# Attention beside the first MLP layer, in token tiles of 256 and 512, on one Trainium2 core

## The chip, the cores and the metric

One core of one Trainium2 chip runs one program. The time is device time in microseconds (us), from the start to the end of the program. Engines are named as in the profile: PE is TensorE (PEld its weight loads), DVE is VectorE, ACT is ScalarE, POOL is GpSimd, and SP is the engine that issues the DMAs.

## The reference

```python
# q, k, v: 4 batches x 8 heads x 576 positions x 64, float32
scores = scale * np.matmul(q, k.transpose(0, 1, 3, 2))
mask = block_i >= block_j            # blocks of 64 positions, causal by block
scores = np.where(mask, scores, -1e9)
attn = np.exp(scores - max) / (sum + 1e-9)
x = (attn @ v) as 2304 tokens x 512
h = x @ w_in;  x = (h * sigmoid(h)) @ w_out            # layer 1: 512 -> 2048 -> 512
h = x @ w_in2; y = (h * sigmoid(1.702 * h)) @ w_out2   # layer 2
```

All is float32. Products of the MLP and the scores are made of three matmuls each: an operand is split into a high part (rounded to fp32r) and a low part (the rest), and lo*hi, hi*hi and hi*lo are summed.

## The kernel before

**Attention** works on 16 head pairs (two heads are one pair; a batch has four pairs). A pair has nine rows, one for each block of 64 queries of both heads; row s has 576 - 64 s keys, the longest first. `scores` (L357 to 373) makes a row with three matmuls, DVE takes its maximum (L643), ACT its exp with the sum (L521), DVE adds 1e-9 to the sums (L602), inverts them (L607) and multiplies the rows (L616). `transposes` (L375 to 392) turns the rows in eight batches into PSUM, which ACT (L496) and DVE (L596) copy out as `pt_sb`; `pv` (L394 to 410) multiplies by v, and `take_pv` (L632) stores the result in `x_f`. The loop holds three pairs at once: rows of pair n, transposes of n - 1, values of n - 2. Operands are prepared ahead: SP loads q, k and v; POOL scales q (L311); ACT makes `k_hi` and `q_hi` (L503, L509); POOL makes `k_lo` (L315) and `q_lo` (L321).

**MLP.** Tokens are cut into three tiles of 768 and both layers run as six tiles of 16 chunks (128 of the 2048 hidden channels each), 96 chunks. `hidden(c)` (L432) makes a chunk's 128 hidden channels, for 512 and then for 256 tokens: 24 matmuls; ACT takes the sigmoid (L554), DVE the product (`gate`, L693), ACT and DVE its high and low part (L561, L697), and `output(c)` (L449) adds the chunk's share to 512 output channels: 24 matmuls. PE issues `hidden(c + 1)` ahead of `output(c)`. The weights of a chunk, 512 KB, are loaded by SP into a ring of two (`w_raw`, L250 to 253) and split by POOL into a ring of four (`w_hi` L329, `w_lo` L331); the split of chunk c waits until `output(c - 4)` is done. ACT and DVE split the next tile's x (L550, L686) and take a tile's output from PSUM (L563, L700).

**Order.** Each engine runs its own list of instructions in program order, and semaphores tie the lists together. All attention comes first; `hidden(0)` sits among the transposes of the last pair (L478 to 482), and the 96 chunks follow (L485). Scores and hidden sums share the four PSUM banks `ps_s`; transposes, values and output sums share `ps_y`.

Of the kernel before, what the change touches and what calls it, by code (L numbers as in the profile page):

```python
# [30 lines left out]
PAIRS = B * H // 2  # L31
# [7 lines left out]
QA = 4  # L39
# [15 lines left out]

GROUPS = [(0, 1), (1, 3), (3, 5), (5, 7), (7, 9)]

SUMS_AT = {1: (4, True), 2: (0, False), 4: (1, False), 6: (2, False), 8: (3, False)}
# [8 lines left out]
TT = 768  # L67
MAIN = 512
SIDE = TT - MAIN
NT = TOK // TT  # L70
NTILES = 2 * NT
NCHUNK = NTILES * NF
RING = 4
ALPHA = (1.0, 1.702)


def build(nc, qT, kT, v_main, v_tail, w_chunks, out):
    ctx = ExitStack()
    with ctx:
# [3 lines left out]
        def sb(stack, name, shape, dt=F32):  # L83
            return stack.enter_context(nc.sbuf_tensor(name, shape, dt))


        x_f = sb(ctx, "x_f", [P, NK * TOK])
        w_hi = sb(ctx, "w_hi", [P, RING, CW], F32R)
        w_lo = sb(ctx, "w_lo", [P, RING, CW], F32R)
        w_raw = sb(ctx, "w_raw", [P, 2, CW])  # L90
        ident = sb(ctx, "ident", [P, P])
        x_hi0 = sb(ctx, "x_hi0", [P, NK, TT], F32R)
        x_lo0 = sb(ctx, "x_lo0", [P, NK, TT], F32R)

        att = ExitStack()
        q_raw = sb(att, "q_raw", [P, 2, S])
        k_raw = (sb(att, "k_raw0", [P, S]), sb(att, "k_raw1", [P, S]))
        q_hi = sb(att, "q_hi", [P, 2, NQ, 2, BLK], F32R)
        q_lo = sb(att, "q_lo", [P, 2, NQ, 2, BLK], F32R)
        scale_sb = sb(att, "scale_sb", [P, S])  # L100
        k_hi = sb(att, "k_hi", [P, 2, S], F32R)
        k_lo = sb(att, "k_lo", [P, 2, S], F32R)
        v_sb = sb(att, "v_sb", [P, 2, NJ, P])
        p_sb = sb(att, "p_sb", [P, 2, PCOLS])

        pt_sb = sb(att, "pt_sb", [P, 2, PT_BLOCKS * P])
        pt_last = sb(att, "pt_last", [P, 2, P])
# [114 lines left out]
        def tokens_of(t):  # L222

            return (t % NT) * TT

# [536 lines left out]
```

## Time and profile before

| what | us |
|---|---|
| median of 3 runs (1039.07 to 1040.92) | 1039.37 |
| profiled execution, its own time | 1041.74 |
| profiled execution, span from first to last instruction | 1040.0 |
| PE busy | 998.6 (96%) |
| PE weight loads busy | 850.5 (82%) |
| DVE busy | 407.0 (39%) |
| ACT busy | 338.8 (33%) |
| POOL busy | 422.3 (41%) |

The profile is of one execution, by the hardware profiler. Busy time is the union of the times of an engine's instructions; PE's weight loads overlap its matmuls, and the ends of matmuls are modelled, so steps between their starts say more than their durations. In the page's 40 slices of 26 us, PE is 50 to 90% busy in the first nine and 90% or more in the rest; DVE goes from 70 to 90% to about 20% at the same place. Of a wait for several semaphores, the profile names the one that came last.

### The profile page before, as it was taken

Reading aid. Unit: us, or ns where it says so; the run is one execution under the profiler, and the core shown is the slowest. Engines: PE = TensorE matmul, PEld = TensorE weight load, DVE = VectorE, ACT = ScalarE, POOL = GpSimd, SP = SyncE. Lnnn points to the kernel's source line nnn. Section 1 sums busy time; section 2 is a strip of 40 time slices with the busy share of each in tenths; the row PEclk is TensorE's granted clock in tenths of the full one; section 3 lists DMA queues with packets and bytes.
Section 4 is the critical chain, followed back from the end, with each engine's and each line's share of the span. In section 5 each row is a group of like instructions: output and inputs, shape, how many; then the busy total and the mean of one; then the engine's idle time right before and its main releaser. Section 6 shows DMA issues by size and latency. Waiting matters only on the chain.

```text
span 1040.0 us, 15291 instructions
## 1 busy us (share of the span) xinstructions
PE 998.6 (96%) x5936; PEld 850.5 (82%) x5936; DVE 407.0 (39%) x777; ACT 338.8 (33%) x652; POOL 422.3 (41%) x261
## 2 busy tenths in 40 slices
PE   5898888889999999999999999999999999999998
PEld 4666666668888888888888888888888888888887
DVE  7978888962222222222322222222232322222222
ACT  5767766652222122222222212222122221212222
POOL 6434443522444444443344444444333444443330
PEclk9989999999999999999999999999999999999999
DMA  4212221030221111112221111111223111131201
GB/s 154 81 46 68 68 68 57 23 101 29 69 69 61 62 61 61 61 61 64 71 70 61 61 61 62 61 61 61 70 72 122 61 61 61 61 122 63 66 34 61
DMA packets 24244, 69.96 MB, mean 67 GB/s; under 512 B 2688, under 2 KB 4224, under 8 KB 24192
## 3 DMA queue, kind: packets, MB, share of 16 engines
q1 hardware_dynamic: 24192, 69.22, 20.6%
q8 instruction: 39, 0.64, 0.3%
q14 instruction: 13, 0.11, 0.0%
HBM read 64.49 MB, written 4.72 MB: 67 GB/s over the span
## 4 chain that ended last, share of the span: by engine, by line
PE 89%; DVE 7%; issue 3%; DVEq 0%; DMA 0%; ACT 0%
PE ps_s L444 13%; PE ps_s L445 13%; PE ps_s L446 13%; PE ps_y L460 8%; PE ps_y L461 8%; PE ps_y L462 8%; PE ps_s L471 4%; PE ps_s L470 4%; PE ps_s L468 4%; PE ps_y L390 4%; PE ps_y L406 4%; PE ps_s L370 4%; DVE den_e L602 2%; DVE nmax L643 2%; DVE p_sb L616 2%
## 5 line engine op out<-in xcount | busy, mean ns | idle before, releaser
L329 POOL CAST w_hi<-w_raw 128x1024 fp32r<-128x1024 f32 x96 | 104.5, 1088 | 472.7 <-PE ps_s L471 452.0
L693 DVE TENSOR_TENSOR g_f<-ps_s,sig 128x768 f32<-128x768 f32 x96 | 91.9, 958 | 497.2 <-ACT sig L554 497.2
L444 PE MATMUL ps_s<-x_hi,w_lo 128*128 128x512 f32 (+1 forms) x768 | 258.9, 337 | 2.5 <-DVE x_f L636 1.5
L445 PE MATMUL ps_s<-x_hi,w_hi 128*128 128x512 f32 (+1 forms) x768 | 259.2, 337 | 0.0
L446 PE MATMUL ps_s<-x_lo,w_hi 128*128 128x512 f32 (+1 forms) x768 | 258.1, 336 | 0.0
L554 ACT ACTIVATE sig<-ps_s 128x768 f32<-128x768 f32 x96 | 78.0, 812 | 503.2 <-PE ps_s L446 503.2
L331 POOL TENSOR_TENSOR w_lo<-w_raw,w_hi 128x1024 fp32r<-128x1024 f32 x96 | 229.8, 2394 | 7.7
L444 PEld LDWEIGHTS ps_s<-x_hi,w_lo 128*128 128x128 f32 x768 | 145.8, 190 | 19.1 <-DVE x_f L636 1.6
L446 PEld LDWEIGHTS ps_s<-x_lo,w_hi 128*128 128x128 f32 x768 | 145.5, 189 | 15.7
L445 PEld LDWEIGHTS ps_s<-x_hi,w_hi 128*128 128x128 f32 x768 | 145.8, 190 | 15.1
L460 PE MATMUL ps_y<-g_hi,w_lo 128*128 128x512 f32 x384 | 150.6, 392 | 0.0
L461 PE MATMUL ps_y<-g_hi,w_hi 128*128 128x512 f32 x384 | 150.6, 392 | 0.0
L462 PE MATMUL ps_y<-g_lo,w_hi 128*128 128x512 f32 x384 | 149.4, 389 | 0.0
L697 DVE TENSOR_TENSOR g_lo<-g_f,g_hi 128x768 fp32r<-128x768 f32 x96 | 92.0, 959 | 87.7 <-ACT g_hi L561 87.7
L561 ACT ACTIVATE g_hi<-g_f 128x768 fp32r<-128x768 f32 x96 | 81.3, 847 | 105.4 <-DVE g_f L693 105.4
L471 PE MATMUL ps_s<-g_lo,w_hi 128*128 128x256 f32 x384 | 108.7, 283 | 0.0
L470 PE MATMUL ps_s<-g_hi,w_hi 128*128 128x256 f32 x384 | 108.6, 283 | 0.0
L468 PE MATMUL ps_s<-g_hi,w_lo 128*128 128x256 f32 x384 | 108.2, 282 | 0.0
L390 PEld LDWEIGHTS ps_y<-ident,p_sb 128*128 128x128 f32 x400 | 46.3, 145 | 59.6 <-DVE pt_last L596 29.2
L390 PE MATMUL ps_y<-ident,p_sb 128*128 128x128 f32 x400 | 72.2, 294 | 23.1 <-DVE pt_last L596 22.8
L521 ACT ACTIVATE p_sb<-ps_s,nmax 128x576 f32<-128x576 f32 (+2 forms) x144 | 75.2, 527 | 41.7 <-DVE nmax L643 41.1
L462 PEld LDWEIGHTS ps_y<-g_lo,w_hi 128*128 128x128 f32 x384 | 72.1, 188 | 15.7
(58 smaller groups left out, 1206.5 us busy)
## 6 DMA issues: line engine op xcount, KB each, us to landing
w_raw<-w_chunks SPq DMA_DIRECT2D x96, 512.0 KB, 3.4
q_raw<-qT SPq DMA_DIRECT2D x16, 288.0 KB, 2.9
k_raw<-kT SPq DMA_DIRECT2D x16, 288.0 KB, 3.1
v_sb<-v_main SPq DMA_DIRECT2D x16, 256.0 KB, 2.5
yT<-x_f SPq DMA_DIRECT2D x2, 1536.0 KB, 7.5
yT<-x_f SPq DMA_DIRECT2D x6, 256.0 KB, 2.1
v_sb<-v_tail SPq DMA_DIRECT2D x16, 32.0 KB, 2.4
```

Source lines behind the costliest of these rows:

```text
L329: nc.gpsimd.tensor_copy(w_hi[:, c % RING, :], w_raw[:, c % 2, :]).then_inc(s_whi, 1)
L331: nc.gpsimd.tensor_tensor(w_lo[:, c % RING, :], w_raw[:, c % 2, :], w_hi[:, c % RING, :].bitcast(F32), ALU.subtract).then_inc(s_w, 1)
L390: last = nc.tensor.transpose(ps_y[:, col:col + P], p_sb[:, par, a:a + P], ident[:, :])
L444: nc.tensor.matmul(dst, lo[:, w], x_hi[t % 2][:, k, a:b], start=(k == 0), stop=False)
L445: nc.tensor.matmul(dst, hi[:, w], x_hi[t % 2][:, k, a:b], start=False, stop=False)
L446: last = nc.tensor.matmul(dst, hi[:, w], x_lo[t % 2][:, k, a:b], start=False, stop=(k == NK - 1))
L460: nc.tensor.matmul(dst, lo[:, w], g1[:, 0:MAIN], start=(f == 0), stop=False)
L461: nc.tensor.matmul(dst, hi[:, w], g1[:, 0:MAIN], start=False, stop=False)
L462: last = nc.tensor.matmul(dst, hi[:, w], g2[:, 0:MAIN], start=False, stop=(f == NF - 1))
L468: nc.tensor.matmul(dst, lo[:, w], g1[:, MAIN:TT], start=(f == 0 and k % 2 == 0), stop=False, skip_group_check=True)
L470: nc.tensor.matmul(dst, hi[:, w], g1[:, MAIN:TT], start=False, stop=False, skip_group_check=True)
L471: last = nc.tensor.matmul(dst, hi[:, w], g2[:, MAIN:TT], start=False, stop=(f == NF - 1), skip_group_check=True)
```

## The change

Attention and the first MLP layer are laid beside each other in all five lists.

- **Tiles.** `LAYER` cuts the tokens into one tile of 256 and four of 512; the second layer takes the four of 512 first and the one of 256 last. There are 160 chunks. x_hi, x_lo, g and the PSUM banks have 512 columns; `ps_h` (hidden, one bank), `ps_a` (attention, three banks) and `ps_y` (output, four banks) are apart.
- **Early part.** The first 256 positions of batch 0 (rows of four blocks, four pairs) are computed first, one pair after the other, with `ps_y` for scores. They are what the first tile needs. The 16 jobs that follow each have rows 4 to 8 of pair n (the upper 320 positions) and, for the first 12 (`FULL`), the four short rows of pair n + 4. The last four have five rows.
- **Windows.** `AT` gives the chunk beside which a job's rows are computed: -1, 3, 7, 11, 14, 18, ... 58. In that chunk PE's list has the rows between pieces of three matmuls of `hidden(c + 1)` and `output(c)`, placed by `WIDE_ROWS` or, beside 256-token chunks, `SLIM_ROWS`. The values of the job before stand at the end of the window's chunk, the job's transposes at the ends of the next two or three chunks. DVE has maxima, two additions, and four multiplications ahead of the window's `gate(c + 1)`; ACT has all exps ahead of the window's sigmoid.
- **Preparation.** In chunk AT + 1 POOL scales the next job's q, at the end of AT + 2 ACT makes its `k_hi` and `q_hi` (`prepare`), and then POOL makes `k_lo` and `q_lo`. A job's buffers p_sb, pt_sb, nmax, den are single, not double.
- **x.** `split_high` and `split_low` make a quarter of the next tile's x behind the values of each job (`PV_AT`).
- **Weights.** POOL splits chunk c + 3 in its step c, now 160 times; in the last tile's chunks (`c >= LAST`) ACT makes the high part and POOL the low part only.

The core of the diff:

```diff
-TT = 768
-MAIN = 512
-SIDE = TT - MAIN
-NT = TOK // TT
-NTILES = 2 * NT
+LAYER = [(0, 256), (256, 512), (768, 512), (1280, 512), (1792, 512)]
+TILES = LAYER + LAYER[1:] + LAYER[:1]
+NTILES = len(TILES)
...
+AT = [-1, 3, 7, 11] + [14 + 4 * n for n in range(JOBS - PER)]
+WINDOW = {c: n for n, c in enumerate(AT)}
+WIDE_ROWS = (0, 0, 3, 3, 3, 4, 5, 5, 6)
+SLIM_ROWS = (0, 0, 4, 4, 5, 7, 7, 8, 8)
+PV_AT = {c: n - 1 for n, c in enumerate(AT) if n}
...
+PREP_AT = {AT[n] + 2: n + 1 for n in range(JOBS - 1)}
+SCALE_AT = {AT[n] + 1: n + 1 for n in range(JOBS - 1)}
...
+            for c in range(-1, NCHUNK):
+                if c + 3 < NCHUNK:
+                    if c + 3 < LAST:
+                        chunk_high(c + 3)
+                    chunk_low(c + 3)
+                if c in SCALE_AT:
+                    scale_q(SCALE_AT[c])
+                if c in PREP_AT:
+                    keys_low(PREP_AT[c])
+                    queries_low(PREP_AT[c])
...
+            for c in range(NCHUNK):
+                n = WINDOW.get(c)
+                before = WIDE_ROWS if TILES[c // NF][1] == TMAX else SLIM_ROWS
+                for piece in range(2 * NK + 1):
+                    if n is not None:
+                        for s in range(rows_of(n)):
+                            if before[s] == piece:
+                                scores(n, s)
+                    if piece < NK:
+                        if c + 1 < NCHUNK:
+                            hidden(c + 1, piece)
+                    elif piece < 2 * NK:
+                        output(c, piece - NK)
+                if c in PV_AT:
+                    values(PV_AT[c], True, n)
+                    if PV_AT[c] < FULL:
+                        values(PV_AT[c], False, n)
+                if c in TRANSPOSE_AT:
+                    for bt in TRANSPOSE_AT[c][1]:
+                        transposes(TRANSPOSE_AT[c][0], bt)
...
+            for c in range(-1, NCHUNK - 1):
+                t, f = c // NF, c % NF
+                if f == 0 and t:
+                    take_output(t - 1)
+                if c > 0 and c in WINDOW:
+                    for s in range(rows_of(WINDOW[c])):
+                        exp_row(WINDOW[c], s)
+                sigmoid(c + 1)
+                g_high(c + 1)
...
+                if c in PREP_AT:
+                    prepare(PREP_AT[c])
...
+                if LAST <= c + 3 < NCHUNK:
+                    chunk_high(c + 3)
...
+                    for s in range(0 if n else 4, min(6, rows_of(n))):
+                        row_max(n, s)
+                    add_guard(n, 0)
+                    if n < FULL:
+                        row_max(n, 6)
+                    invert(n, 0)
+                    multiply(n, 0)
+                    if n < FULL:
+                        row_max(n, 7)
+                        row_max(n, 8)
+                    multiply(n, 1)
+                    multiply(n, 2)
+                    add_guard(n, 1)
+                    invert(n, 1)
+                    multiply(n, 3)
+                    gate(c + 1)
+                    if c in PV_AT:
+                        take_upper(PV_AT[c])
+                    g_low(c + 1)
```

## Rows read from the trace of the kernel before

**Rows 1.** Busy time by engine: attention, MLP, tail (PEclk is the granted clock).

```profile
7.95:237.98 230.03, 199.92 (x1353) 145.77 (x1353) 191.52 (x544) 152.44 (x419) 97.99 (x67) 0.97 0.22 67
237.98:1036.62 798.64, 798.64 (x4584) 704.66 (x4584) 210.29 (x227) 181.98 (x228) 320.12 (x184) 1.00 0.20 65
1036.62:1040.00 3.38, 0.00 (x1) 0.00 (x0) 0.69 (x1) 0.00 (x0) 0.00 (x0) 1.00 0.73 256
```

Columns: from:to, length, then busy us (and instructions) of PE, PEld, DVE, ACT and POOL, granted clock, DMA share, GB/s.

**Rows 2.** The page's chain that ended last, by engine.

```profile
PE 89%; DVE 7%; issue 3%; DVEq 0%; DMA 0%; ACT 0%
```

**Rows 3.** Busy time by engine over one head pair in mid-attention.

```profile
99.77:113.19 13.42, 11.60 (x85) 8.32 (x84) 11.75 (x33) 9.28 (x27) 5.71 (x4) 1.00 0.22 66
```

**Rows 4.** Timeline of PE in `hidden(0)`: start, duration, engine, line, operation.

```profile
225.60 0.40 PE L444 MATMUL ps_s<-x_hi,w_lo 128*128 128x512 f32 x1
...
227.65 0.28 PE L444 MATMUL ps_s<-x_hi,w_lo 128*128 128x256 f32 x1
...
228.96 0.28 PE L446 MATMUL ps_s<-x_lo,w_hi 128*128 128x256 f32 x1
```

**Rows 5.** Instructions by line and shape, DVE in attention: busy us, mean ns, idle before.

```profile
L616 DVE TENSOR_SCALAR p_sb<-p_sb,rden 128x192 f32<-128x192 f32 x16 | 21.2, 1322 | 0.0
...
L643 DVE TENSOR_REDUCE nmax<-ps_s 128x1 f32<-128x256 f32 x16 | 6.4, 402 | 1.2 <-PE ps_s L370 1.2
...
L616 DVE TENSOR_SCALAR p_sb<-p_sb,rden 128x256 f32<-128x256 f32 x16 | 5.5, 343 | 0.0
...
L616 DVE TENSOR_SCALAR p_sb<-p_sb,rden 128x64 f32<-128x64 f32 x16 | 3.9, 243 | 0.0
```

**Rows 6.** The same view: ACT's batch copy and keys, POOL's low parts.

```profile
L496 ACT ACTIVATE pt_sb<-ps_y 128x512 f32<-128x512 f32 x80 | 47.4, 592 | 32.7 <-PE ps_y L390 32.7
...
L321 POOL TENSOR_TENSOR q_lo<-q_raw,q_hi 64x576 fp32r<-64x576 f32 x30 | 43.1, 1435 | 2.7
...
L315 POOL TENSOR_TENSOR k_lo<-k_raw,k_hi 128x576 fp32r<-128x576 f32 x15 | 21.4, 1424 | 100.4 <-ACT k_hi L503 99.7 <-DVE k_lo L667 0.7
...
L503 ACT ACTIVATE k_hi<-k_raw 128x576 fp32r<-128x576 f32 x16 | 11.0, 688 | 1.1 <-DMA k_raw<-kT 1.1
```

**Rows 7.** Timeline of DVE and POOL from 101 us.

```profile
101.04 0.68 DVE L643 TENSOR_REDUCE nmax<-ps_s 128x1 f32<-128x512 f32 x1
...
101.36 2.96 POOL L321 TENSOR_TENSOR q_lo<-q_raw,q_hi 64x576 fp32r<-64x576 f32 x2
...
101.64 1.15 DVE L602 TENSOR_SCALAR den_e<-den 128x2 f32<-128x2 f32 x1
...
102.70 1.73 DVE L616 TENSOR_SCALAR p_sb<-p_sb,rden 128x256 f32<-128x256 f32 x2
```

**Rows 8.** Instructions by line, POOL's split of a weight chunk.

```profile
L329 POOL CAST w_hi<-w_raw 128x1024 fp32r<-128x1024 f32 x96 | 104.5, 1088 | 472.7 <-PE ps_s L471 452.0
...
L331 POOL TENSOR_TENSOR w_lo<-w_raw,w_hi 128x1024 fp32r<-128x1024 f32 x96 | 229.8, 2394 | 7.7
```

**Rows 9.** Timeline of ACT: its two table loads, and the first sigmoid.

```profile
0.74 1.28 ACT L532 ACT_TABLE_LOAD   x1 [0.74 <-PEq L756]
...
232.23 1.28 ACT L554 ACT_TABLE_LOAD   x1
...
233.52 0.81 ACT L554 ACTIVATE sig<-ps_s 128x768 f32<-128x768 f32 x1
```

**Rows 10.** DMA issues of the page: KB each, us to landing.

```profile
w_raw<-w_chunks SPq DMA_DIRECT2D x96, 512.0 KB, 3.4
```

**Rows 11.** Busy time and granted clock of two stretches of 4 us.

```profile
46.00:50.00 4.00, 2.19 (x16) 1.40 (x15) 4.00 (x11) 1.51 (x5) 2.88 (x3) 1.00 0.32 86
50.00:54.00 4.00, 4.00 (x23) 2.55 (x21) 2.64 (x11) 3.16 (x10) 0.00 (x0) 0.64 0.17 66
```

**Rows 12.** Timeline of POOL and DVE at the start.

```profile
5.39 1.79 POOL L311 TENSOR_TENSOR q_raw<-q_raw,scale_sb 128x576 f32<-128x576 f32 x1 [2.12 <-DMA q_raw<-qT]
...
5.96 1.84 DVE L667 TENSOR_TENSOR k_lo<-k_raw,k_hi 128x576 fp32r<-128x576 f32 x1
```

More of the change, by code:

```diff
@@ L95, in build @@
[L95 to L104, printed above, removed]
@@ L412, in pair @@
-            def pair(n, par, it, cur=True, prev=True, prev2=True, also=None):
-                for s in range(NQ):
-                    if cur:
-                        scores(n, par, it, s)
-                    if prev2:
-                        for part in MULTIPLY.get(s, ()):
-                            pv(n - 2, par, it - 1, part)
-                    if prev and s in TRANSPOSE:
-                        transposes(n - 1, 1 - par, TRANSPOSE[s])
-                    if also and s in also:
-                        also[s]()
@@ L478, in first_hidden @@
[L478 to L488 removed]
+            early_transposes(0)
+            early_scores(2)
@@ new lines, in _ @@
+            early_transposes(1)
+            early_values(0)
+            early_scores(3)
+            early_transposes(2)
+            early_values(1)
+            early_transposes(3)
+            scores(0, 0)
+            scores(0, 1)
+            early_values(2)
+            early_values(3)
+            scores(0, 2)
+            scores(0, 3)
+            for k in range(NK):
+                hidden(0, k)
+                scores(0, 4 + k)
+            scores(0, 8)
+            pe.wait_ge(s_pad, 1)
@@ L578, in _ @@
-            act.wait_ge(s_xe, 2 * H)
-            pair(PAIRS, 0, PAIRS // 2, cur=False, ahead=False, also={k: (lambda k=k: split_x(0, k)) for k in range(NK)})
-            for c in range(NCHUNK):
+                    nc.scalar.activation(x_kt[:, k, a:a + w], bank_y(k)[:, 0:w], ACT.Copy).then_inc(s_ea, 1)
+            for a in range(2):
+                early_high(a)
+            early_exp(0)
+            early_high(2)
+            early_exp(1)
+            early_high(3)
+            early_take(0)
@@ new lines, in _ @@
+            for r in range(LB):
+                early_multiply(PER - 1, r)
+            early_take(3)
+            row_max(0, 0)
+            early_values(2)
+            row_max(0, 1)
+            split_low(0, 0)
+            split_low(0, 1)
+            early_values(3)
+            for i in range(LB, NQ, 2):
+                last = nc.vector.memset(p_sb[:, POFF[i] + BLK * (i + 1):POFF[i] + PAD[i]], 0.0)
+            last.then_inc(s_pad, 1)
+            row_max(0, 2)
+            split_low(0, 2)
```

1026 lines of the change are left out of this document (602 added, 424 removed).

## The prediction

> **What bounds the kernel now.** I first read the stretches [rows 1]. Of a span of 1040.0 us, TensorE (PE) is busy 199.92 in the 230.03 us of attention and all 798.64 in those of the two MLP layers. The reader is to see two regimes: from 237.98 on nothing but less work for PE can shorten the kernel; before that some 30 us of PE idle time are to be had, beside the 7.95 us ahead of its first matmul. Then the chain that ended last [rows 2]: 89% PE, 7% DVE. Then one head pair in the middle of attention [rows 3]: of 13.42 us PE is busy 11.60, DVE 11.75, ACT 9.28, POOL 5.71. Attention is a relay among four engines in which DVE and PE are both nearly full. In the MLP stretch DVE, ACT and POOL are busy 26%, 23% and 40%: room for attention, and PE's idle time would be filled by matmuls.
>
> **PE's work after the change.** A 512-column matmul takes (227.65 - 225.60)/9 = 0.228 us, a 256-column one (228.96 - 227.65)/11 = 0.119 [rows 4]. Before, each of 96 chunks has 24 of each: 8.33 us, 800 in all. After, 128 chunks have 24 of 512 columns (5.48 us) and 32 have 24 of 256 (2.86): 792.8 us, 7.4 less, since fewer narrow matmuls are issued. A pair costs 11.6 us [rows 3], of which 4.6 are scores and 3.6 values by the steps between their starts. I keep 11.6 between MLP matmuls; the lower bound is 10.8, without the gaps of 0.15 to 0.2 us at changes of kind, worth 13 us over 16 pairs; the upper one 11.6, as that includes all gaps.
>
> **Head, up to `hidden(1)`.** The four early jobs go through a serial chain: scores, maximum, exp, sums, multiply, transpose, take, values. Per job DVE has four maxima (0.402 for 256 columns), four multiplications (0.24 to 0.34 [rows 5]), low parts, sums, two copies: 4.6 us, plus waits for each exp; from a first score at 6 us the four end near 27. Then job 0's nine rows, the splits of x, and 4 multiplications stand ahead of `gate(0)`: `hidden(1)` at 40 us. PE does 4 x 3.4 us for the early jobs and 6.4 for job 0 meanwhile. Bounds 34 and 47 us (each early job 1.5 us shorter or longer).
>
> **Rest of PE's work.** 16 x 11.6 = 185.6, less 13.6 and 6.4, is 166 us; MLP 792.8 less `hidden(0)` is 791.4; the tail 3.4 us [rows 1], 3.2 with copies of 256. Without any stall: 40 + 166 + 791.4 + 3.2 = 1000.6. The kernel can give away 39 us before it is level, so what counts is the hand-offs.
>
> **Operands of the next job late.** At the end of chunk AT+2 ACT takes batch 4 (0.59), then makes k_hi (0.69 for 576 columns, 0.96 for the 832 of a wide job); then POOL makes k_lo (1.42, so 2.05) and q_lo (2 x 1.44) [rows 6]. With hand-overs of 0.4 in all that is 6.9 us from the end of PE's chunk AT+2 to the next job's first score. PE has one chunk meanwhile. In the 256-token tile that is 2.86 + 0.6 of transposes: a stall of 3.5, three times. Job 4 is prepared in chunk 13 and its window is 14: 6.8 us. With 512 tokens PE has 6.1: 0.8, seven times. The last four jobs have shorter operands: none. Sum 17.3 + 5.6 = 22.9; bounds 12 and 30 (chain shorter or longer by a third of a chunk).
>
> **DVE behind POOL.** POOL starts two q_lo subtractions at 101.36; DVE's addition on two numbers per partition, issued at 101.64, takes 1.15 us, and the next two multiplications 1.73, until POOL is done [rows 7]. The means say the same: 192 columns take 1.322 us, 256 columns 0.343 [rows 5]. So a DVE op from SBUF to SBUF waits for POOL's op to end; the reduction from PSUM at 101.04 does not (0.68). Ahead of `gate(c+1)`, on which `hidden(c+2)` waits, DVE now has two such additions and four multiplications. In a 512-token window I lay the rows end to end: PE ends the last score at 8.7 us, the output at 10.0 (5.48 + 4.6) and the values at 13.7; DVE ends its multiplications at 10.9, ACT its last exp at 9.5 and the sigmoid at 11.4, and the gate ends at 12.3. POOL's chunk (1.09 + 2.39 [rows 8]) lies before 7 us or after 10. Slack 1.4 us: 3 us over eleven windows. In the 256-token tile POOL comes out of q_lo two chunks in arrears and works through the multiplications without pause; six ops meet parts of 2.39 us ops, and the gate comes some 3 us after PE: 4 x 3 = 12. Together 15; bounds 0 (DVE always gets in first) and 15 windows x 2.39 = 36.
>
> **Activation tables.** Exp and Sigmoid are a load of 1.283 us apart, so thirty more loads [rows 9]. The load to Exp falls where ACT idles: the first one ran at 0.74, ahead of the wait for its data. The load to Sigmoid stands behind the window's last exp (9.5 to 10.8 above): hidden by the 1.4 us of slack, price 0.
> In the trace the sigmoid starts 0.01 us after its load (232.23 + 1.28, 233.52). The Trainium skill (ScalarE: Activation LUTs, What ACT_TABLE_LOAD costs) speaks against the change: a drain of 1380 ns comes with each switch, 2.66 us in all. By it, as an estimate from that page, each sigmoid would come 1.4 us later and the sum would rise by 0 to 10 us; the trace shows no such drain, so none is taken.
>
> **x split at tile borders.** `hidden` of chunks 16, 32 and 48 needs the last job's x, which DVE splits only behind all multiplications of the window: 2.5 + 2.9 + 2.9 = 8.3 by the same laying end to end; bounds 0 and 12.
>
> **Last tile.** Landing 3.4 us [rows 10], the cast now on ACT about 1.08 (1024 columns by the slope of its copies [rows 6]), w_lo 2.39, hand-overs 0.2: 7.1 us around a ring of two slots, 3.5 per chunk where PE wants 2.86. Over some 11 chunks 7.5 us; ACT can't run on the four buffers' lead, as the cast waits in its queue ahead of the next sigmoid. Bounds 0 (lead used) and 12.
>
> **Clock.** After 4 us with PE busy 2.19, the granted clock was 0.64 for the next 4 [rows 11]: 1.4 us lost. Four stalls of 3.5 to 7 us may each bring the lower of the two levels (1.2 instead of 2.4 GHz). I take 2 us in all; bounds 0 and 8.
>
> **SP's queue.** Windows put q, k and v loads between chunk loads; chunk loads run two chunks ahead of POOL's need, which hides them. Price 0; if that cover goes, one landing, 3.4 us, per window.
>
> **Sum.** 1000.6 + 22.9 + 15 + 8.3 + 7.5 + 2 = 1056.3 us of span. The profiled execution took 1041.74 with its span of 1040.0; the median of the runs is 1039.37, 0.6 below that span. So 1056 us, 1.6% slower.
>
> **Rivals.** 1, the other side: the hand-offs in chunks 0 to 15 are absorbed. Place: windows 3, 7, 11, 14 and their gates. Price: 17.3 for late operands and 12 for POOL's hold on DVE, with them the clock's 2, and 6 of the last tile if its lead is used: 1056 - 37 = 1019. It decides where all stalls together stay below 39. For it: the 256-column multiplication at 102.70 did get in between two POOL ops. Against it: the chain of 6.9 us is made of plain durations. Chance 0.28.
> 2, worse: DVE is also held in the 512-token windows, and not in its multiplications alone, but in subtractions of two SBUF operands (`g_low`, `split_low`): at 5.96 such a k_lo took 1.84 us beside POOL's scaling [rows 12]. One 2.39 us op more in some nine windows: 1056 + 22 = 1078. Chance 0.14.
> The Trainium skill (SBUF — State Buffer, SBUF: two separate sides) states the hold for both kinds of operation, as an exclusive lock; by that rule, the trace agrees.
> 3, the change does less than it says: attention runs beside the MLP, but parts of each stall give the gain back to the level of before, within 2 us of 1039. Chance 0.04.
>
> **Numbers.** Forecast 0.54, with 1044 to 1068 as its own range. The whole range takes in rival 1's value and rival 2's: 1020 to 1078. A measurement of this kernel tells some 0.2% from no change. Faster 0.28, same 0.04, slower 0.68.
>
> **What would show it.** `hidden(1)` near 40 us; chunk 16 at 165 (126 us for 94 of PE work); chunk 62 at 551; then 5.48 us per chunk; chunks 144 to 159 at 3.5. Scores at chunks 3, 7, 11, 14 wait for q_lo, and multiplications there average over 1 us. I am wrong if PE is over 97% busy between 40 and 551 us, or if the last tile runs at 2.86 per chunk.

## The result, and the profile after

The kernel after takes 1061.14 us (median of 4 runs, 1057.68 to 1065.3), the one before 1039.22 beside it (1038.38 to 1040.92). The ratio is 1.0211, with a 95% interval of 1.017 to 1.0251: slower by 22 us where 17 were forecast. The profiled execution took 1057.68 us with a span of 1055.7; it is the fastest of the four. Medians are of executions that took the usual time: one of the kernel before (1966.74 us) and one of the run with four edits together (5532.26 us) are left out.

First the page of the kernel after: busy time by engine, then the chain that ended last, by engine [rows 2].

```profile
PE 985.9 (93%) x5168; PEld 825.6 (78%) x5168; DVE 466.1 (44%) x878; ACT 422.4 (40%) x837; POOL 649.8 (62%) x386
...
PE 80%; POOL 7%; DVE 6%; ACT 3%; DMA 2%; issue 2%; POOLq 0%; DVEq 0%
```

The chain had no POOL before; now 7% of it is POOL, which makes operands that PE waits for. Next the stretches of the kernel after, cut where `hidden(1)` starts, at chunks 16 and 62, and ahead of the last tile, with the columns of [rows 1].

```profile
0.00:54.20 54.20, 31.61 (x157) 25.50 (x158) 39.26 (x88) 23.81 (x75) 29.52 (x31) 0.84 0.41 130
54.20:181.90 127.70, 99.66 (x717) 91.89 (x716) 75.55 (x164) 63.59 (x146) 77.47 (x47) 0.91 0.31 104
181.90:552.90 371.00, 361.86 (x1961) 294.31 (x1959) 199.51 (x397) 188.63 (x374) 227.97 (x137) 1.00 0.27 91
552.90:997.80 444.90, 444.90 (x1969) 368.74 (x1970) 132.06 (x196) 119.07 (x198) 281.62 (x160) 1.00 0.30 102
997.80:1055.70 57.90, 47.90 (x373) 45.19 (x371) 19.67 (x34) 27.33 (x47) 33.25 (x14) 1.00 0.41 144
```

Against the forecast, stretch by stretch. The forecast's column is added from the prediction's terms, without its 2 us for the clock, for which it gives no place:

| stretch | forecast | measured | difference |
|---|---|---|---|
| up to `hidden(1)` | 40 | 54.2 | +14.2 |
| chunks 0 to 15 | 126 | 127.7 | +1.7 |
| chunks 16 to 61 | 385.7 | 371.0 | -14.7 |
| chunks 62 to 143 | 448.1 | 444.9 | -3.2 |
| last tile and tail | 55.0 | 57.9 | +2.9 |

The span came out 0.6 us from the forecast's 1056.3 because two errors of some 14 us cancel; that closeness is luck. PE idles 22.6 us in the first stretch, 28.0 in the second, 9.1 in the third, none in the fourth and 10.0 in the fifth. What it waited for, in the whole trace after: total, times, longest.

```profile
PE ps_a L557 <- POOL q_lo L428: 20.9, 11, 6.0
PE ps_a L513 <- DVE p_sb L850: 14.5, 7, 4.9
PE ps_h L620 <- DVE g_f L908: 9.6, 4, 2.9
PE ps_h L620 <- POOL w_lo L443: 6.5, 9, 1.2
PE ps_y L498 <- POOL k_lo L408: 5.2, 1, 5.2
PE ps_h L620 <- DVE x_lo L900: 3.3, 2, 2.4
PE ps_h L620 <- issue: 2.8, 1, 2.8
```

The reader is to see the forecast's terms by name. Late operands are the first line (15.6 of it in four waits in chunks 0 to 15, 5.3 in seven of at most 0.8 later). DVE behind POOL, ahead of the gate, is the third and the last: three waits of 2.9 us in the windows of chunks 3, 7 and 11, and the 2.8, which is the same wait in the window of chunk 14 (DVE's gate ended at 175.30, 0.1 us ahead of the matmul at 175.40). The fourth wait of that third line, 1.0 us up to 53.95, belongs to the head: PE waits there for `gate(0)`. The last tile is the fourth. The second, DVE's multiplications in the early jobs (L850), was in no term.

DVE by form, with the columns of [rows 5]: in chunks 0 to 15 of the kernel after the multiplication of 512 columns, then `g_low` and `gate` in chunks 16 to 61, then `g_low` behind them:

```profile
L882 DVE TENSOR_SCALAR p_sb<-p_sb,rden 128x512 f32<-128x512 f32 x4 | 9.0, 2243 | 0.0
...
L913 DVE TENSOR_TENSOR g_lo<-g_f,g_hi 128x512 fp32r<-128x512 f32 x47 | 48.1, 1023 | 25.1 <-ACT g_hi L758 25.1
...
L908 DVE TENSOR_TENSOR g_f<-ps_h,sig 128x512 f32<-128x512 f32 x46 | 31.7, 690 | 82.3 <-ACT sig L750 82.3
...
L913 DVE TENSOR_TENSOR g_lo<-g_f,g_hi 128x512 fp32r<-128x512 f32 x81 | 56.1, 692 | 56.6 <-ACT g_hi L758 56.6
```

A multiplication of 512 columns takes 2.24 us in the first tile and 0.48 later. `g_low`, with both operands in SBUF, takes 1.02 us beside attention and 0.69 without; `gate`, of the same size with an operand in PSUM, takes 0.69 in both. One instance of each, begun while POOL was at work:

```profile
207.14 2.38 POOL L443 TENSOR_TENSOR w_lo<-w_raw,w_hi 128x1024 fp32r<-128x1024 f32 x1
...
208.53 1.53 DVE L913 TENSOR_TENSOR g_lo<-g_f,g_hi 128x512 fp32r<-128x512 f32 x1
...
225.35 3.45 POOL L428 TENSOR_TENSOR q_lo<-q_raw,q_hi 64x576 fp32r<-64x576 f32 x2
225.45 0.69 DVE L908 TENSOR_TENSOR g_f<-ps_h,sig 128x512 f32<-128x512 f32 x1 [3.04 <-ACT sig L750]
```

That `gate` simply never met POOL can be ruled out in the same trace. Of its operations of 512 columns in chunks 16 to 143, 84 began inside a running operation of POOL, with 0.19 to 1.35 us of it to go, and each took 0.69. Of the 46 of `g_low` in chunks 16 to 61, the 20 that began inside one, with 0.73 to 0.99 us of it to go, took 1.28 to 1.54; the other 26 took 0.69. Behind chunk 61 `g_low` began inside none, which is why it takes 0.69 there.

One window of the first tile in the kernel after, in the timeline:

```profile
68.06 0.40 PE L557 MATMUL ps_a<-k_hi,q_lo 128*128 128x288 f32 x1 [3.51 <-POOL q_lo L428]
...
77.72 2.44 POOL L443 TENSOR_TENSOR w_lo<-w_raw,w_hi 128x1024 fp32r<-128x1024 f32 x1
...
78.20 3.75 DVE L882 TENSOR_SCALAR p_sb<-p_sb,rden 128x512 f32<-128x512 f32 x2
...
80.25 0.38 ACT L750 ACTIVATE sig<-ps_h 128x256 f32<-128x256 f32 x1
...
82.61 0.42 DVE L908 TENSOR_TENSOR g_f<-ps_h,sig 128x256 f32<-128x256 f32 x1
...
83.17 0.55 PE L620 MATMUL ps_h<-x_hi,w_lo 128*128 128x256 f32 x1 [2.87 <-DVE g_f L908]
```

Both forecast waits are here: 3.51 us for the operands (3.5 forecast), and 2.87 for the gate (3 forecast). The sigmoid was done at 80.6; the gate came 2 us later because two multiplications took 3.75 us between POOL's operations.

### The profile page after: what moved, and what is told of

Read it like the earlier page. It is cut to its first block, busy times and chain, and to the rows that moved or that the text cites. A ratio compares the mean times of both kernels' runs of the same rounds, so it can differ in the third digit from the quotient of the medians.

```text
span 1055.7 us, 13667 instructions
## 1 busy us (share of the span) xinstructions
PE 985.9 (93%) x5168; PEld 825.6 (78%) x5168; DVE 466.1 (44%) x878; ACT 422.4 (40%) x837; POOL 649.8 (62%) x386
## 4 chain that ended last, share of the span: by engine, by line
PE 80%; POOL 7%; DVE 6%; ACT 3%; DMA 2%; issue 2%; POOLq 0%; DVEq 0%
PE ps_h L620 12%; PE ps_h L621 11%; PE ps_h L622 11%; PE ps_y L636 11%; PE ps_y L638 11%; PE ps_y L637 11%; PE ps_a L557 6%; POOL q_lo L428 3%; PE ps_a L602 3%; PE ps_a L579 3%; POOL k_lo L420 2%; DMA w_raw<-w_chunks 2%; DVE p_sb L882 2%; DVE p_sb L850 1%; POOL w_lo L443 1%
## 5 line engine op out<-in xcount | busy, mean ns | idle before, releaser
L443 POOL TENSOR_TENSOR w_lo<-w_raw,w_hi 128x1024 fp32r<-128x1024 f32 x160 | 386.2, 2414 | 39.6 <-ACT w_hi L763 28.0
L620 PE MATMUL ps_h<-x_hi,w_lo 128*128 128x512 f32 (+1 forms) x640 | 244.0, 381 | 22.2 <-DVE g_f L908 9.6
L622 PE MATMUL ps_h<-x_lo,w_hi 128*128 128x512 f32 (+1 forms) x640 | 237.9, 372 | 0.0
L636 PE MATMUL ps_y<-g_hi,w_lo 128*128 128x512 f32 (+1 forms) x640 | 237.4, 371 | 0.5 <-DVE g_lo L913 0.5
L621 PE MATMUL ps_h<-x_hi,w_hi 128*128 128x512 f32 (+1 forms) x640 | 237.8, 371 | 0.0
L638 PE MATMUL ps_y<-g_lo,w_hi 128*128 128x512 f32 (+1 forms) x640 | 236.2, 369 | 0.0
L637 PE MATMUL ps_y<-g_hi,w_hi 128*128 128x512 f32 (+1 forms) x640 | 236.0, 369 | 0.0
L913 DVE TENSOR_TENSOR g_lo<-g_f,g_hi 128x512 fp32r<-128x512 f32 (+1 forms) x160 | 126.1, 788 | 95.6 <-ACT g_hi L758 95.2
L620 PEld LDWEIGHTS ps_h<-x_hi,w_lo 128*128 128x128 f32 x640 | 122.9, 192 | 46.9 <-issue 14.8
L621 PEld LDWEIGHTS ps_h<-x_hi,w_hi 128*128 128x128 f32 x640 | 123.0, 192 | 18.9
L636 PEld LDWEIGHTS ps_y<-g_hi,w_lo 128*128 128x128 f32 x640 | 121.3, 190 | 20.2 <-DVE g_lo L913 0.7
L557 PE MATMUL ps_a<-k_hi,q_lo 128*128 128x288 f32 (+8 forms) x144 | 47.8, 332 | 22.8 <-POOL q_lo L428 20.9
```

Source lines behind the costliest of these rows:

```text
L443: nc.gpsimd.tensor_tensor(w_lo[:, c % RING, :], w_raw[:, c % 2, :], w_hi[:, c % RING, :].bitcast(F32), ALU.subtract).then_inc(s_w, 1)
L557: last = nc.tensor.matmul(dst, q_part[:, par, i, :, :].rearrange("p h c -> p (h c)"), k_part[:, par, a:a + width], start=(q_part is q_lo), ...
L620: nc.tensor.matmul(dst, lo, x_hi[:, t % 2, k, 0:w], start=(k == 0), stop=False)
L621: nc.tensor.matmul(dst, hi, x_hi[:, t % 2, k, 0:w], start=False, stop=False)
L622: last = nc.tensor.matmul(dst, hi, x_lo[:, t % 2, k, 0:w], start=False, stop=(k == NK - 1))
L636: nc.tensor.matmul(dst, lo, g_hi[:, c % 2, 0:w], start=(f == 0), stop=False)
```

## The experiments

All times of stretches below come from the first instruction of a chunk's sigmoid on ACT in the timeline: from the start of the span to that of chunk 1, then to 16, to 63, to 144, and from there to the end of the span. A run's median is the time of the kernel as a whole.

```
                          median   0-1    1-16   16-63  63-144  144-end
after                     1061.1   55.7   124.1  376.1  439.4   60.5
multiplications on ACT    1054.4   50.5   124.2  378.0  439.4   60.4
operands one earlier      1049.4   55.2   114.0  378.4  439.4   60.2
three raw slots           1054.6   55.9   123.2  377.7  439.3   56.7
gate ahead                1073.2   55.7   138.0  378.3  439.4   60.2
exp for sigmoid           1060.5   54.8   129.7  377.7  439.4   60.5
slots and cast first      1056.2   55.5   128.3  378.0  439.3   53.2
matmuls in the head       1065.3   55.1   126.7  378.0  439.4   64.5
three together            1040.0   49.2   112.0  378.4  439.3   56.7
four together             1034.8   50.4   112.1  378.4  439.3   52.1
sums first                1033.6   48.9   112.7  378.4  439.4   52.0
x split moved             1030.8   47.0   112.1  378.4  439.3   52.0
```

**The early multiplications on ACT.** Sixteen operations leave DVE.

```diff
-            def early_multiply(a, r):
-                if r == 0:
-                    dve.wait_ge(s_eden, 2 * a + 2)
-                nc.vector.tensor_scalar(e_probs(a, r), e_probs(a, r), e_rden[:, a, r:r + 1], None,
-                                        ALU.mult).then_inc(s_enm, 1)
...
+            def early_multiply(a):
+                act.wait_ge(s_eden, 2 * a + 2)
+                for r in range(LB):
+                    nc.scalar.activation(e_probs(a, r), e_probs(a, r), ACT.Copy,
+                                         scale=e_rden[:, a, r:r + 1]).then_inc(s_enm, 1)
```

> The sixteen multiplications of the early part move from DVE to ACT; nothing else changes. Theory (DVE is held by POOL's ops): the change's head lasts 54 us instead of the 40 forecast, and its DVE multiplications took 0.6 to 2.3 us each where 0.24 to 0.34 is their own time; ACT is not held, so the head shortens by about 10 us and the kernel with it (1061 to about 1051). Rival (the head is a serial relay at the lower clock): ACT's multiplications are each a little longer than DVE's own, so the head stays within 2 us of 54 and the kernel within 2 us.

Measured: 1054.4 us, ratio 1.0138 (1.0097 to 1.0179); the sigmoid of chunk 1 starts at 50.5 us instead of 55.7. In the kernel after, DVE and POOL in the head (timeline):

```profile
15.60 2.34 POOL L443 TENSOR_TENSOR w_lo<-w_raw,w_hi 128x1024 fp32r<-128x1024 f32 x1
...
15.86 2.20 DVE L850 TENSOR_SCALAR p_sb<-p_sb,e_rden 128x192 f32<-128x192 f32 x1
...
27.89 2.34 POOL L443 TENSOR_TENSOR w_lo<-w_raw,w_hi 128x1024 fp32r<-128x1024 f32 x1
...
27.95 2.33 DVE L850 TENSOR_SCALAR p_sb<-p_sb,e_rden 128x64 f32<-128x64 f32 x1
...
34.10 4.74 DVE L850 TENSOR_SCALAR p_sb<-p_sb,e_rden 128x256 f32<-128x256 f32 x4
```

Even 64 columns take 2.33 us, and end with POOL's operation. With them on ACT, PE's wait there is 5.7 us in three, for ACT's batch copies, in place of 14.5. So the hold is real in the head too, but this way gave 5 us of the 10 expected: a relay was behind it (below). The four executions of this run lie 8.6 us apart, so the stretch (5.2 us) says more than the total (6.7).

**Operands one chunk earlier.**

```diff
-PREP_AT = {AT[n] + 2: n + 1 for n in range(JOBS - 1)}
-SCALE_AT = {AT[n] + 1: n + 1 for n in range(JOBS - 1)}
+PREP_AT = {AT[n] + 1: n + 1 for n in range(JOBS - 1)}
+SCALE_AT = {AT[n]: n + 1 for n in range(JOBS - 1)}
```

> Scaling q and preparing the next job's operands stand one chunk earlier in POOL's and ACT's lists (AT and AT + 1 instead of AT + 1 and AT + 2). Theory (late operands): PE's waits for q_lo ahead of a job's scores, 15.6 us in chunks 0 to 15 and 5.3 us later, go; with the lower clock behind them, 15 to 22 us less: about 1042. Rival (POOL is the bound of the 256-token tile, 3.5 us a chunk and 6.4 a job): the wait only moves to the weight split or to the gates, and the kernel stays within 5 us of 1061.

Measured: 1049.39 us, ratio 1.009 (1.0073 to 1.0107), 12 us less, between the 15 to 22 of the theory and the 5 of the rival. PE's waits in its trace:

```profile
PE ps_a L557 <- DVE pt_sb L887: 7.3, 10, 1.3
PE ps_h L620 <- DVE g_f L908: 7.2, 4, 2.6
...
PE ps_a L602 <- ACT p_sb L725: 5.1, 3, 1.8
...
PE ps_a L557 <- POOL q_lo L428: 1.3, 1, 1.3
```

The wait for q_lo fell from 20.9 to 1.3 us. In chunks 1 to 16 that gave 10.1 us. There the wait for q_lo had been 15.6, but PE's idle time fell by 7.2 only (28.0 to 20.8), as waits for ACT's exps (5.1) and a weight split (1.7) came in its place; the other 3 us are PE's matmuls, busy 93.2 instead of 96.1 us at a granted clock of 0.96 instead of 0.90. In chunks 16 to 63 it gave nothing, since the ten waits of 7.3 us for DVE's batch copies took the place of the 5.3 that left.

**Three slots for the raw weights.** `w_raw` and its semaphores get three slots instead of two; SP waits for `s_w` two chunks back instead of one.

```diff
-                if c >= 2:
-                    sp.wait_ge(s_w, c - 1)
+                if c >= RAW:
+                    sp.wait_ge(s_w, c - RAW + 1)
```

> The ring for unsplit weights gets a third slot, the loads run one chunk further ahead. Theory (the last tile goes round a two-slot ring of landing, ACT cast and POOL low part, 7.1 us for two chunks): chunks 144 to 159 go from 3.55 to about 2.9 us, 8 to 10 us less: about 1052; the layers between stay at 5.44 us a chunk. Rival (the cast in ACT's list, between the high part of g and the next sigmoid, sets the pace): the last tile stays at 3.4 us or more per chunk, and the kernel within 2 us of 1061.

Measured: 1054.57 us, ratio 1.0126 (1.0098 to 1.0155). PE's wait for w_lo in the last tile of the kernel after stands above (6.5 us in nine); ACT's for the landing there:

```profile
ACT w_hi L763 <- DMA w_raw<-w_chunks: 6.9, 11, 1.8
```

With three slots ACT's cast waits for no transfer there, and PE for POOL only this much (L621 and L444 are the L620 and L443 of the kernel after):

```profile
PE ps_h L621 <- POOL w_lo L444: 2.0, 7, 0.3
```

The last stretch is 3.8 us shorter, 3.29 us per chunk (between the sigmoids of 145 and 159) instead of 3.56. So the landing was part of the ring, as forecast, but the 2.9 us expected did not come: it did not set the pace alone.

**Three slots, and the cast ahead of the sigmoid.** The rest of that ring was ACT's cast, which stands behind sigmoid and g_high.

```diff
+                if LAST <= c + 3 < NCHUNK:
+                    chunk_high(c + 3)
                 sigmoid(c + 1)
                 g_high(c + 1)
...
-                if LAST <= c + 3 < NCHUNK:
-                    chunk_high(c + 3)
```

> The raw ring of three, and in the last tile ACT's cast of chunk c + 3 stands ahead of the sigmoid of c + 1 instead of behind the high part of g. With the ring alone the last tile went from 3.55 to 3.29 us a chunk. Theory (what is left is the way cast, then POOL's low part 2.40, then the hidden matmuls two chunks on, begun 2 us too late): 2.9 us a chunk, 5 us less than with the ring alone, about 1049. Rival (POOL's low part and the loads' landing set 3.3): no change from the ring alone, 1054.

Measured: 1056.18 us, ratio 1.0136 (1.0101 to 1.0171): by the total, no gain over three slots alone. By the stretches there is one: 53.2 us instead of 56.7, and 2.91 us per chunk, PE's own pace. In this profiled execution chunks 1 to 16 took 5.1 us more, which the edit does not touch (see the clock, below). The total, where 1049 was expected, hid a gain that the stretch shows.

**The gate ahead of the multiplications** in the windows of the first tile.

```diff
+                elif n and t == 0:
+                    for s in range(rows_of(n)):
+                        row_max(n, s)
+                    gate(c + 1)
+                    take_upper(PV_AT[c])
+                    g_low(c + 1)
+                    take_lower(PV_AT[c])
+                    for g in range(3):
+                        add_guard(n, g)
+                        invert(n, g)
+                        for s in range(3 * g, 3 * g + 3):
+                            multiply(n, s)
```

> In the four windows of the 256-token tile DVE does the nine maxima, then the gate, the copies of the values and the low part of g, and only then the additions, inversions and multiplications. Theory (DVE is held by POOL in multiplications that stand ahead of the gate): PE's 9.6 us of waits for g_f in these windows go, and the kernel is about 8 us shorter: 1053. Rival (the sigmoid is late, behind nine exps and a table load): the waits stay, now behind the sigmoid, and the multiplications, now later, delay the transposes: within 2 us of 1061 or slower.

Measured: 1073.21 us, ratio 1.0315 (1.0297 to 1.0332), 12 us slower than the kernel after. The timeline of this run at the window shown above, and at the gate behind it:

```profile
80.53 0.36 PE L620 MATMUL ps_h<-x_hi,w_lo 128*128 128x256 f32 x1 [0.16 <-DVE g_f L908]
...
84.03 3.65 DVE L882 TENSOR_SCALAR p_sb<-p_sb,rden 128x384 f32<-128x384 f32 x3
...
89.76 0.56 PE L620 MATMUL ps_h<-x_hi,w_lo 128*128 128x256 f32 x1 [5.13 <-DVE g_f L908]
```

The wait of 2.87 us is gone, and one of 5.13 stands at the next gate, behind the same multiplications. Between the sigmoids of chunks 1 and 16 PE idles 37.1 us instead of 28.0; the other 4.8 us of the 13.9 lost are PE's own, busy 100.9 instead of 96.1 at a granted clock of 0.86 instead of 0.90. DVE's held time did not become slack in this order.

**Exp in the place of Sigmoid beside attention.** Up to chunk 59 the kernel computes exp(h) where the reference has a sigmoid, so no table is loaded there.

```diff
-                nc.scalar.activation(sig[:, 0:w], ps_h[:, 0:w], ACT.Sigmoid,
+                nc.scalar.activation(sig[:, 0:w], ps_h[:, 0:w], ACT.Exp if c <= AT[-1] + 1 else ACT.Sigmoid,
```

> In chunks 0 to 59, beside attention, ACT applies Exp where it applied Sigmoid, so the thirty activation table loads between them go; the kernel computes another function there, all else is the same. Theory (the loads lie in idle time of ACT or within slack): at most 4 us less than 1061, nearly all in the 256-token tile. Rival (each load costs its 1.28 us, or 2.66 with a drain, on the path to the gate): 15 windows, so 15 to 35 us less.

Measured: 1060.48 us, ratio 1.0184 (1.0163 to 1.0205), against 1061.14 and 1.0211. ACT's table loads in the kernel after, and below them those of this run:

```profile
L750 ACT ACT_TABLE_LOAD x16 | 20.5, 1283 | 0.3
...
L725 ACT ACT_TABLE_LOAD x15 | 19.2, 1283 | 0.3
```

```profile
L750 ACT ACT_TABLE_LOAD x1 | 1.3, 1283 | 0.0
```

Thirty loads, 38.5 us of ACT's time, cost the kernel nothing that can be told: the sigmoid of the window above started at 78.98 instead of 80.25 us, and the gate still had to wait for DVE. In the windows with 512 tokens the window's sigmoid comes 1.4 us earlier and the next one not at all: from chunk 22's to 23's and on to 24's the steps are 13.51 and 6.69 us, and 14.94 and 5.27 in the kernel after, 20.2 both times. That is the slack that the forecast counted on.

**Matmuls in the head.** Ninety matmuls of 256 columns are added, whose results nothing reads, so that PE does not idle in the early jobs.

```diff
+            def fill(a, count):
+                if a == 3 and count:
+                    pe.wait_ge(s_exe, 1)
+                for _ in range(count):
+                    nc.tensor.matmul(ps_h[:, 0:LT] if a == 3 else bank(2)[:, 0:LT],
+                                     q_hi[:, 1, 0, :, :].rearrange("p h c -> p (h c)"),
+                                     k_hi[:, 1, 0:LT], start=True, stop=True)
+            FILL = {(1, 6): 16, (1, 7): 6, (2, 6): 12, (2, 7): 18, (3, 6): 36, (3, 7): 2}
...
+                    fill(a, FILL.get((a, bt), 0))
```

> Ninety matmuls of 256 columns into a PSUM bank that nobody reads are put where PE waits in the early part (ahead of the transposes of early jobs 1 to 3); about 10 us of PE work at 2.4 GHz, in waits of 13 us. Theory (the lower clock is half of the head's lateness: granted 0.84 over 0 to 54 us, and the scores and values of each early job are links of the serial chain): clock near 1.00 and hidden(1) 4 to 7 us earlier. Rival (DVE's and POOL's operations set the head, PE's speed doesn't): hidden(1) within 1 us of 54.2, or later by what the filling delays.

Measured: 1065.26 us, ratio 1.0221 (1.0188 to 1.0254). Two stretches of the head in the kernel after, and the same two with the matmuls:

```profile
30.00:38.00 8.00, 2.78 (x13) 1.67 (x14) 5.69 (x8) 0.00 (x0) 7.71 (x6) 0.50 0.17 66
38.00:46.00 8.00, 7.00 (x32) 4.65 (x31) 3.24 (x7) 1.90 (x5) 0.59 (x1) 0.55 0.01 3
```

```profile
30.00:38.00 8.00, 7.18 (x61) 6.50 (x59) 6.11 (x8) 0.00 (x0) 7.77 (x6) 0.99 0.19 66
38.00:46.00 8.00, 6.78 (x38) 4.87 (x36) 3.96 (x9) 2.42 (x7) 0.79 (x1) 0.79 0.02 4
```

The granted clock rose from 0.50 to 0.99 and from 0.55 to 0.79, and the sigmoid of chunk 1 came only 0.6 us earlier, as the rival had it. So the lower clock in the early jobs goes with the long head and does not make it. It was not lifted everywhere: job 0's first scores ran at the lower level with the matmuls too (0.50 from 41.5 to 43.0 us; 512-column steps of 0.43 us, for the 0.228 worked out from [rows 4]), and what that costs was not tried. The total is 4 us above that of the kernel after because of stretches that the edit does not touch: the last took 64.5 us instead of 60.5, with 9.3 us of waits for w_lo instead of 6.5.

**Three together** (multiplications on ACT, operands earlier, three slots).

> The early multiplications on ACT, operands prepared one chunk earlier and the raw ring of three, together. Theory (three separate losses, one behind another in time): the gains of the single runs add, 1061 - 7 - 12 - 6 = about 1036, level with or just below the kernel before. Rival (they stand on one resource, POOL, and each cure shifts wait to the next): less than half of the sum, 1048 or more.

Measured: 1040.01 us (10 runs, 1037.9 to 1040.42), ratio 0.9989 (0.9979 to 1.0). The three alone took 6.7, 11.8 and 6.6 us off 1061.14, together 21.1 of their 25.1. The stretches, less noisy, say the same: 5.2 in the head, 10.1 in chunks 1 to 16 and 3.8 in the last, each alone, and 6.5, 12.1 and 3.8 together. So the waits are largely separate, and the change without them is level with the kernel before.

**Four together**, with the cast ahead of the sigmoid, and **the sums first** in the early jobs:

```diff
+                early_sums(a)
                 if a >= 2:
                     early_values(a - 2)
-                early_sums(a)
                 if a:
                     early_take(a - 1)
```

> The three edits of the run before it (multiplications of the early jobs on ACT, operands prepared one chunk earlier, three raw slots for the weights) and the fourth, the last tile's cast of chunk c+3 ahead of the sigmoid of chunk c+1. Theory: in the trace with three slots the stretch from the sigmoid of chunk 144 to the end took 56.7 us, with the cast ahead of the sigmoid 53.2, though the total of that run did not show it, as the stretches before it were slower there; so 3.5 us less than the 1040.0 of the three together, 1036.5 us, ratio to the kernel before 0.9955 to 0.9975, and 2.9 us per chunk in the last tile. Rival: the cast holds up ACT's sigmoids by as much as it gains, the two runs of the last tile agree in their totals because nothing was gained: 1040 us, ratio 0.999.

> The four edits, and in the early jobs DVE's sum and reciprocal stand ahead of its copy of the values of two jobs before, instead of behind it. In the trace of the three together ACT finished the exponentials of the third early job at 18.5 us, but its multiplications began at 21.35, since DVE waited 3.85 us for the values of an earlier job, that copy being ahead of the sum in its queue; so again at 26.4. Theory: what made the head longer than forecast is this order, a relay in which each early job waits for the values of an earlier one: 2.3 us less for each of two early jobs, some 4.5 in all, first sigmoid at 42 us instead of 46.5, total 1032 us, ratio about 0.992. Rival: POOL's operands for the first full job (its last subtraction ended at 27.6 us) or its weight splits set the head: the first sigmoid stays above 45 us and the total within 1.5 us of the run with four edits.

Measured, four together: 1034.77 us, ratio 0.9934 (0.9922 to 0.9947); the last stretch took 52.1 us, so here the cast shows in the total as well. Sums first: 1033.64 us, ratio 0.9926 (0.9913 to 0.9939), 1.1 less where 4.5 were expected; chunk 1's sigmoid came 1.5 us earlier. The first sigmoid, that of chunk 0, came at 44.9 us, neither at 42 nor above 45, and the total is the rival's. DVE's last early batch copy and the x splits in the timeline of three together, then of sums first:

```profile
31.46 0.42 DVE L860 COPY pt_sb<-ps_a 128x256 f32<-128x256 f32 x1 [3.28 <-PE ps_a L514]
...
37.40 2.60 DVE L905 TENSOR_TENSOR x_lo<-x_f,x_hi 128x256 fp32r<-128x256 f32 x2
```

```profile
25.90 0.42 DVE L859 COPY pt_sb<-ps_a 128x256 f32<-128x256 f32 x1 [1.76 <-PE ps_a L514]
...
32.77 3.69 DVE L904 TENSOR_TENSOR x_lo<-x_f,x_hi 128x256 fp32r<-128x256 f32 x2
...
38.21 2.12 DVE L904 TENSOR_TENSOR x_lo<-x_f,x_hi 128x256 fp32r<-128x256 f32 x1
```

The relay did give its 5.6 us (31.46 to 25.90). Of these, 1.8 went to a new wait for POOL's q_lo (first score at 27.70), and the first matmul of `hidden(0)` came 4.8 us earlier (35.05 for 39.81). But the x splits now fell beside POOL's weight splits and its scaling of q: 3.69 us for two, of which PE waited 1.24, and 2.12 for the last, where a free one takes 0.40, and the maxima of the later rows stand behind that one. The first sigmoid kept 1.5 of the 4.8.

**The x split moved.** Part 0 stands ahead of the first full row's maximum, part 1 behind it, part 3 is read from PSUM, and ACT's exp of the first full row moves behind its high part of part 1 (not shown in the lines).

```diff
             early_take(3)
+            split_low(0, 0)
             row_max(0, 0)
+            split_low(0, 1)
             early_values(2)
             row_max(0, 1)
-            split_low(0, 0)
-            split_low(0, 1)
...
-            split_low(0, 3)
+            split_low(0, 3, e_out(3))
```

> The run with the sums first, and in the head DVE splits the first tile's x in other places: part 0 ahead of the first full row's maximum, part 1 behind it (they stood together behind the second row's maximum), ACT's high part of part 1 one row earlier, and part 3 reads the values from PSUM, where PE wrote them, instead of their copy in SBUF. In the trace with the sums first DVE took 3.69 us for parts 0 and 1 (POOL in its weight splits and its scaling of q from 32.25 to 37.35) and 2.12 for part 3, where a free one takes 0.40. Theory: POOL's hold on DVE's operations of two SBUF operands has taken back the 5.6 us that the relay gave, and an operand in PSUM frees the operation of it: part 3 takes 0.45 us, the two others no longer stand ahead of a maximum, the first matmul of hidden(0) starts at 34 us instead of 35.05, the first sigmoid at 42 instead of 44.9, total 1031 us, ratio about 0.990. Rival: an operand in PSUM makes no difference, as the other operand and the output are in SBUF: part 3 takes about 2 us again, the first sigmoid stays above 44 us and the total within 1 us of 1033.6.

Measured: 1030.82 us, ratio 0.9909 (0.9893 to 0.9926), the theory's 1031, the fastest of all and 9 us faster than the kernel before. DVE and POOL in its timeline:

```profile
36.15 1.24 POOL L437 CAST w_hi<-w_raw 128x1024 fp32r<-128x1024 f32 x1
...
36.88 0.41 DVE L905 TENSOR_TENSOR x_lo<-ps_y,x_hi 128x256 fp32r<-128x256 f32 x1
...
37.46 2.36 POOL L444 TENSOR_TENSOR w_lo<-w_raw,w_hi 128x1024 fp32r<-128x1024 f32 x1
...
37.94 1.91 DVE L877 TENSOR_SCALAR den_e<-den 128x3 f32<-128x3 f32 x1
```

Part 3 took 0.41 us, begun and ended within POOL's cast; 1 us later an addition on three numbers waited 1.91 us for the end of POOL's subtraction. The first matmul of `hidden(0)` came at 35.31 rather than at the 34 expected, and chunk 1's sigmoid at 47.0, that of chunk 0 at 43.0 instead of 42. One operation does not show that PSUM was what freed it, and parts 0 and 1 changed their places as well; how the 1.9 us of the first sigmoid divide among the three changes was not tried. That an operand in PSUM frees an operation of two inputs rests on the 84 of `gate` above.

## Why the prediction was right, and where it was wrong

**The total and the sign** were right, 1056 for 1061.1, and so was the mechanism of the likeliest case: the work fits beside the MLP, and the hand-offs cost more than the 39 us that the kernel can give away. The closeness of the total is in part luck: with its head at 54 us and the rest as forecast the sum would have been 1070. Rival 1 fell: the waits of windows 3, 7, 11 and 14 were not absorbed. Of rival 2 a part is there: `g_low` in the wide tiles was held (1.02 us for 0.69), yet no gate in chunks 16 to 61 made PE wait. Of the signs named, PE is 92% busy from 40 to 551 us (471.4 of 511.0), under the 97 that would have refuted it; multiplications in the first tile were to average over 1 us, and the 41 of chunks 0 to 15 average 0.73, as only the three longest rows of a window are held. Taken out of the path one by one, the waits bring the change from 2.1% slower to 0.9% faster, so the sign hung on them.

**Head, up to `hidden(1)`: the term that failed.** 40 us forecast, bounds 34 and 47, 54.2 measured. The step counted four multiplications per early job at 0.24 to 0.34 us, from the free ones in [rows 5]. The sixteen took 16.7 us in all (1.573, 1.022, 0.834 and 0.757 on average for 192, 64, 128 and 256 columns, four of each), against some 4.6 when free: 12 us of DVE's time too little. Not all of it lay on the path: with the sixteen on ACT the head was 5.2 us shorter. The prediction had DVE's hold by POOL in hand, from [rows 7], and charged it in the windows, but not in the head, where POOL splits chunks 0 to 3 and prepares job 0 without pause from 13.8 to 38.6 us. With those multiplications on ACT, the sums ahead of the copies and the x splits moved, 8.7 of the 14 us were won back (55.7 to 47.0). What is left, some 5 us, was not taken apart; the part of the clock in it is open (see the matmuls in the head).

**Rest of PE's work.** Chunks of 512 columns take 5.44 us, not 5.48, 5 us over 128 chunks. The 14.7 us that chunks 16 to 61 came short of the forecast are 9.4 of PE's work (361.9 busy; the forecast's 385.7 less its 14.4 of stalls is 371.3) and 5.3 of stalls that did not come (9.1 idle). Of the 9.4, 1.8 are the pace of 46 chunks. The rest is attention. A window of nine rows adds 11.5 us to its four chunks (239.7 - 206.4 between the sigmoids of 19 and 23 is 33.3, less 4 x 5.44 = 21.8), 0.8 of which is PE's wait for q_lo, so 10.7 of work, where the forecast kept 11.6 and had 10.8 as its lower bound: some 6 us over the seven such windows. The four windows of five rows add 7.7 each (529.2 - 499.7 = 29.5). The 11.6 was attention by itself with its gaps between kinds of work, the 10.8 without them; that beside the MLP these gaps are filled fits, but was not looked at one by one.

**Operands of the next job late.** 17.3 forecast in the first tile, 15.6 measured; 5.6 behind it, 5.3 measured. Moving the preparation removed nearly all of this wait, so the chain was read rightly; half of the time went to other waits (above).

**DVE behind POOL.** 12 forecast for the first tile, 8.6 + 2.8 = 11.4 measured at the four gates named, and 1.0 at `gate(0)` in the head; 3 in the wide windows, 0 measured.

**Activation tables.** 0 forecast; without the thirty loads the kernel takes as long as with them. The page of the Trainium skill weighed there (ScalarE: Activation LUTs, What ACT_TABLE_LOAD costs) would have had each sigmoid come another 1380 ns later; the trace after shows it at 80.25 us, right behind the load of 78.96 + 1.28, which itself starts 0.02 us behind the last exp (78.74 + 0.20). The measurement decides.

**x split at tile borders.** 8.3 forecast, 3.3 measured, in two waits.

**Last tile.** 3.5 us per chunk forecast, 3.56 measured, 7.5 us over PE's pace forecast against 8.4 won by three slots and the earlier cast (60.5 to 52.1). Both parts of the ring named there, landing and cast in ACT's queue, are shown by the edits that take them out of it.

**Clock.** 2 us forecast. It is more, and it varies (below). In chunks 0 to 15 PE was busy 99.7 us where the terms have 94, at a granted clock of 0.91, and idle 28.0 where they have 32: the 127.7 for 126 is again two errors that cancel. The four runs of the kernel after lie 7.6 us apart, those of the kernel before 2.5. That the clock spreads them is not shown run by run: the slowest of the four (1065.3) has the lowest clock, 0.968, but 1062.34 goes with 0.984 and 1057.68 with 0.981.

**The rival with its point of decision** (39 us of stalls) was the right way to ask. PE's idle time in the kernel after is 69.8 us (1055.7 less 985.9), and 45.9 in the fastest version (1028.8 less 982.9).

## What to carry to other kernels

Work that moves beside an engine's full-time job brings its hand-offs with it: add up what one can give away (here 39 us), and put every wait of the new places against that sum, the start of the kernel too, since a mechanism found in the steady part acts as well where the pipeline fills. When one engine holds another, a change of order can just move the wait (the gate ahead: 12 us slower); look for a third engine for the operation (ACT here), an operand in PSUM, or a time at which the other engine is idle. When a total doesn't show a gain, compare the stretch that the edit touches before dropping it: the earlier cast showed nothing alone and 5 us with the others.

## What the runs showed of the hardware

**POOL holds DVE's smallest operations.** An addition on three numbers per partition, 0.15 us by itself, took 1.91 us in the run with the x split moved, and two multiplications took 3.75 while POOL did two operations in a row. The Trainium skill (SBUF — State Buffer, SBUF: two separate sides) calls the shared ports an exclusive lock, which the second to come waits out; the trace agrees, with 2.33 us for 64 columns beside a POOL operation of 2.34. An operation of two inputs, one of them in PSUM, is not held: 84 of `gate` took 0.69 us inside POOL's.

**The granted clock varies between executions at the same place.** The run with three slots and the one with slots and cast first are the same program up to the last tile. Their stretches from 54 to 184 us:

```profile
54.00:184.00 130.00, 100.69 (x725) 92.49 (x725) 76.26 (x166) 64.32 (x148) 80.17 (x48) 0.91 0.33 105
```

```profile
54.00:184.00 130.00, 101.02 (x699) 93.16 (x699) 74.94 (x162) 62.81 (x144) 76.77 (x46) 0.87 0.33 108
```

With PE's idle time the same to within 1 us, chunks 1 to 16 took 123.2 us at a granted clock of 0.91 and 128.3 at 0.87; the kernel after has 124.1 at 0.91, the run with exp for sigmoid 129.7 at 0.86. So about 1 us for each hundredth, and 5 us by chance alone. In the stage where PE always has work the clock was 1.00 in each trace, and chunks 63 to 144 took 439.3 or 439.4 us in all twelve. That PE's gaps bring the lower clock is shown for the early jobs: filling them raised it from 0.50 to 0.99, and eight matmuls of values at 31 us, 1.55 us in the kernel after and in each of the five other runs with the same early part, took 0.87; in the first tile it fits that the clock rose from 0.90 to 0.96 when the operands came earlier and the idle time fell from 28.0 to 20.8 us. A granted clock of 1.00 can also be a gap in the record: the run with operands one earlier shows 1.00 from 0 to 54 us, yet took those 1.55 us, the pace of the lower level, for the same eight matmuls.
